# Setting the bound register of an indirect scatter before the semaphore wait, and waiting at the scatter itself

## The chip, the cores and the metric

The kernel runs on one core of one Trainium2 chip. The metric is the device time of one execution in microseconds (us). Its engines are PE (TensorE), DVE (VectorE), ACT (ScalarE), POOL (GpSimd) and SP (SyncE); each has a sequencer that reads its own list of instructions, written PEq, DVEq, ACTq, POOLq and SPq in the profile.

## What is computed

Three stages follow each other. The first is a linear attention with decay, the second an ELU network of 1536 tokens x 384 features with 2048 hidden units, the third a top-1 mixture of 8 experts with 384 places each. Cut to what matters:

```
x = attention(r, k, v, w, u)                 # 1536 x 384
h = x @ w_in; x = where(h > 0, h, exp(min(h, 0)) - 1) @ w_out
e = argmax(x @ w_gate); gate_w = softmax(x @ w_gate)[e]
disp[e, n_e] = x[i]                          # tokens sorted by expert
y = maximum(disp @ w1[e], 0) @ w2[e]
out[i] = gate_w[i] * y[e, n_e]               # back to the token's row
```

## The kernel before, in words

All products run on PE in fp32r, each value split into a high and a low part, so that one product is three matmuls (L1362 to L1364). ACT and DVE bring results out of the banks and form the parts; POOL forms many of the low parts (L707 for the ELU network's `g_lo`, L724 for half of each expert's weights).

Tokens are sorted by expert through memory. The ELU network works on 6 blocks (NB) of 256 tokens (two tiles of 128). When a block is done, DVE computes the slot number of each token (`slot_i`, L1150, which raises the semaphore `s_row`), and POOL writes the block's two tiles to the tensor `slots` with two indirect DMAs (`scatter_rows`, L681 to L685): 12 scatters in the whole run. They stand in POOL's list between the `g_lo` operations (L707) and the pieces of the attention that POOL works ahead on; the last two stand behind a wait for the first loads of the experts.

SP loads each expert's 256 rows back (`xrow`). An expert runs 8 steps on PE, and its output is two tiles of 128 tokens x 384, scaled by the gate on DVE (`yrow`, L1254 and L1314, which raise `s_ye`). `tok_i` (L1308, `s_tok`) holds the row of `out` to which each token goes. POOL sends each tile there with an indirect DMA (L729 in `scatter_tile`): 16 scatters, of which the first two, the next two (`scatter_out(0, 1)`), eight in a loop over the middle experts, and four behind the loop. The last expert's second tile is the last result of the run. Afterwards SP waits until all scatters have landed (L557), each engine reads a number that tells whether an expert had more than 256 tokens (L558, L758), and all engines meet (L177).

Of the kernel before, what the change touches and what calls it, by code (L numbers as in the profile page):

```python
# [12 lines left out]
def build(nc, B, H, S, D, DFF, NE, FE, CAP, rkt_in, nat_in, decay, bonus, bonus_pair, win, wout, wouttr, wgate, wexp, out, slots):  # L13
    T = B * S
# [44 lines left out]
    NSLOT = LATE + CAP  # L59
# [117 lines left out]
    with ctx:  # L177
# [13 lines left out]
        def pair(name):  # L191
            return [sem(f"{name}{p}") for p in range(2)]
# [88 lines left out]
        s_ye = pair("ye_ready")  # L281
        s_tok = pair("tok_ready")
# [292 lines left out]
        def _(pool):  # L575
# [98 lines left out]
            one = pool.alloc_register("one")  # L674
            last_slot = pool.alloc_register("last_slot")
            last_token = pool.alloc_register("last_token")
            pool.reg_mov(one, 1)

            def scatter_rows(n, t):

                pool.wait_ge(s_row, n + 1)  # L681
                pool.reg_add(last_slot, one, NSLOT - 2)  # L682
                nc.gpsimd.indirect_dma_start(
                    out=slots, out_offset=bass.IndirectOffsetOnAxis(ap=slot_i[n % 2][:, t:t + 1], axis=0),
                    in_=x2row[n % 2][:, t, NE:NE + XR], in_offset=None, bounds_check=last_slot, oob_is_err=False).then_inc(s_scat[n % 2], 16)  # L685
# [15 lines left out]
            for n in range(NB):  # L701
                for f in range(FT):
                    q = FT * n + f
                    if q == FT * NB - 1:
                        break
                    pool.wait_ge(s_ghi, q + 1)
                    nc.gpsimd.tensor_tensor(g_lo[:, f % 4, :], elu[:, f % 2, :], g_hi[:, f % 4, :].bitcast(F32),  # L707
                                            ALU.subtract).then_inc(s_glo, 1)
                    ahead(n, f)
                    at = f - route(n - 1)["scatter"]  # L710
                    if n and 0 <= at < BT:
                        if n == 1 and at == 0:
                            pool.wait_ge(s_blank, 16 * NBLANK)
                        scatter_rows(n - 1, at)
            pool.wait_ge(s_xr[0], 32)
            for t in range(BT):
                scatter_rows(NB - 1, t)

            def split_w2(e_i, r):

                for c in range(N1):
                    pool.wait_ge(s_ehi[r], 2 * N1 * e_i + N1 + c + 1)
                    cols = slice(W1 + c * ECH, W1 + (c + 1) * ECH)
                    nc.gpsimd.tensor_tensor(EL[r][:, cols], ER[r][:, cols], EH[r][:, cols].bitcast(F32),  # L724
                                            ALU.subtract).then_inc(s_elo2[r], 1)

            def scatter_tile(r, t):
                pool.reg_add(last_token, one, T - 2)  # L728
                nc.gpsimd.indirect_dma_start(  # L729
                    out=out, out_offset=bass.IndirectOffsetOnAxis(ap=tok_i[r][:, t, :], axis=0),  # L730
                    in_=yrow[r][:, t, :], in_offset=None, bounds_check=last_token,
                    oob_is_err=False).then_inc(s_sout[r], 16)

            def scatter_out(i, r):
                pool.wait_ge(s_tok[r], i + 1)
                for t in range(2):
                    pool.wait_ge(s_ye[r], 2 * i + t + 1)
                    scatter_tile(r, t)

            split_w2(0, 1)  # L740
            pool.wait_ge(s_atok, 1)
            pool.wait_ge(s_ye[0], 1)
            scatter_tile(0, 0)
            pool.wait_ge(s_tok[0], 1)
            pool.wait_ge(s_ye[0], 2)
            scatter_tile(0, 1)
            split_w2(1, 0)
            scatter_out(0, 1)
            with pool.Fori(1, NE // 2 - 1) as i:
                split_w2(i, 1)  # L750
                scatter_out(i, 0)
                split_w2(i + 1, 0)
                scatter_out(i, 1)
            split_w2(NE // 2 - 1, 1)
            scatter_out(NE // 2 - 1, 0)
            scatter_out(NE // 2 - 1, 1)
            pool.wait_ge(s_over, 1)
            over = pool.value_load(n_over[0:1, 0:1], min_val=0, max_val=T)  # L758
            with pool.If(over > SN):
# [1110 lines left out]
```

## Time and profile before

| | |
|---|---|
| median of 3 runs | 415.98 us |
| lowest and highest run | 415.86, 416.11 us |
| span of the profiled execution | 413.8 us |
| what lies around the span (median less span) | 2.1 us |
| PE busy | 406.2 us, 98% of the span |
| POOL busy | 231.0 us, 56% |
| DVE busy | 243.7 us, 59% |
| PE's share of the chain that ended last | 92% |
| POOL's share of it | 1% |

The profiled execution has no time of its own beside its span; what lies around the span is taken from the median. The span runs from the first to the last instruction. A row of the time line has its start, its duration and the instruction; in brackets stands how long the engine was idle before it, and what ended that. Instructions of a sequencer (a register, a semaphore wait, a branch) don't count as busy time and show in the chain of waits and in the view of their line, not in the time line of the engine.

### The profile page before, as it was taken

To read this page: it belongs to the slowest core of one execution; us is meant where nothing else is said; L and a number is where in the kernel's file an instruction comes from. 1 tells how busy PE (TensorE), PEld (TensorE's weight loads), DVE (VectorE), ACT (ScalarE), POOL (GpSimd) and SP (SyncE) were. 2 spreads that over 40 slices of the span, in tenths; PEclk is the share of its full clock that TensorE was granted. 3 is DMA by queue.
4 is the path that set the end of the run, shared out by engine and by line. 5 is a ranking of instruction groups with operands and counts; after the bars stand their busy time and mean duration, and the time that the engine had idled before them with its cause. 6 is when DMAs were issued, how large, how long until landed. Compare 5 with 4: busy or idle time off the path is not lost.

```text
span 413.8 us, 9451 instructions
## 1 busy us (share of the span) xinstructions
PE 406.2 (98%) x3697; PEld 390.8 (94%) x3697; DVE 243.7 (59%) x576; ACT 188.1 (45%) x409; POOL 231.0 (56%) x239
## 2 busy tenths in 40 slices
PE   8999999999999999999999999999999999999994
PEld 8799799999999999999999999999999999999994
DVE  7787955376576547654653487785635556364521
ACT  4786543233433333333343555553645445464420
POOL 3789775467856685668234336075073461825531
PEclk9999999999999999999999999999999999999999
DMA  7998996204030403020018001827383845729000
GB/s 287 402 396 351 367 344 243 82 38 148 12 119 2 139 21 118 3 86 21 2 20 344 2 2 38 326 77 248 125 308 101 340 160 203 295 89 360 5 31 28
DMA packets 18650, 64.98 MB, mean 157 GB/s; under 512 B 2203, under 2 KB 11717, under 8 KB 16432
## 3 DMA queue, kind: packets, MB, share of 16 engines
q1 hardware_dynamic: 16672, 59.67, 39.5%
q0 software_dynamic: 1792, 4.73, 3.0%
q8 instruction: 28, 0.46, 0.4%
q14 instruction: 14, 0.11, 0.1%
q10 hardware_dynamic: 144, 0.00, 0.0%
HBM read 51.98 MB, written 13.21 MB: 158 GB/s over the span
## 4 chain that ended last, share of the span: by engine, by line
PE 92%; DVE 4%; issue 1%; POOL 1%; ACT 1%; DMA 0%; POOLq 0%; DVEq 0%
PE bank L1362 27%; PE bank L1364 26%; PE bank L1363 26%; PE bank L1383 2%; PE bank L1412 1%; PE bank L1448 1%; PE bank L1452 1%; PE bank L1686 1%; PE bank L1441 1%; PE bank L1444 1%; PE bank L1539 1%; PE bank L1721 1%; PE bank L1722 1%; PE bank L1725 1%; PE bank L1625 1%
## 5 line engine op out<-in xcount | busy, mean ns | idle before, releaser
L707 POOL TENSOR_TENSOR g_lo<-elu,g_hi 128x256 fp32r<-128x256 f32 x95 | 73.8, 778 | 86.5 <-ACT g_hi L875 86.3
L1362 PE MATMUL bank<-xt,wd_hi 128*128 128x256 f32 x285 | 80.7, 283 | 0.6 <-DVE elu L1190 0.6
L1364 PE MATMUL bank<-xt,wd_lo 128*128 128x256 f32 x285 | 80.5, 282 | 0.0
L1363 PE MATMUL bank<-xt,wd_hi 128*128 128x256 f32 x285 | 80.4, 282 | 0.0
L866 ACT ACTIVATE elu<-elu 128x256 f32<-128x256 f32 x96 | 40.1, 418 | 76.5 <-DVE elu L1182 75.9
L1362 PE MATMUL bank<-wd_hi,g_hi 128*128 128x392 f32 (+1 forms) x192 | 67.5, 352 | 0.0
L1364 PE MATMUL bank<-wd_hi,g_lo 128*128 128x392 f32 (+1 forms) x192 | 65.3, 340 | 0.0
L1363 PE MATMUL bank<-wd_lo,g_hi 128*128 128x392 f32 (+1 forms) x192 | 65.2, 339 | 0.0
L1190 DVE SCALAR_TENSOR_TENSOR elu<-elu,bank 128x256 f32<-128x256 f32 x96 | 40.3, 420 | 40.5 <-ACT elu L866 40.5
L875 ACT CAST g_hi<-elu 128x256 fp32r<-128x256 f32 x96 | 39.0, 406 | 45.0 <-DVE elu L1190 45.0
L1362 PEld LDWEIGHTS bank<-xt,wd_hi 128*128 128x128 f32 x285 | 54.0, 189 | 1.3 <-DVE elu L1190 1.1
L1364 PEld LDWEIGHTS bank<-xt,wd_lo 128*128 128x128 f32 x285 | 54.2, 190 | 0.0
L1363 PEld LDWEIGHTS bank<-xt,wd_hi 128*128 128x128 f32 x285 | 54.1, 190 | 0.0
L1294 DVE SCALAR_TENSOR_TENSOR ge_lo<-bank,ge_hi 128x256 fp32r<-128x256 f32 x56 | 23.8, 425 | 48.8 <-ACT ge_hi L933 48.8
L1182 DVE TENSOR_SCALAR elu<-bank 128x256 f32<-128x256 f32 x80 | 33.8, 423 | 31.1 <-PE bank L1364 26.5
L933 ACT ACTIVATE ge_hi<-bank 128x256 fp32r<-128x256 f32 x56 | 21.6, 385 | 53.1 <-PE bank L1364 31.1
L724 POOL TENSOR_TENSOR wd_lo<-wd_raw,wd_hi 128x1024 fp32r<-128x1024 f32 x12 | 30.4, 2556 | 26.7 <-ACT wd_hi L946 24.3
L1362 PEld LDWEIGHTS bank<-wd_hi,g_hi 128*128 128x128 f32 x192 | 36.4, 189 | 2.0 <-issue 1.4
L1363 PEld LDWEIGHTS bank<-wd_lo,g_hi 128*128 128x128 f32 x192 | 36.4, 190 | 0.0
L724 POOL TENSOR_TENSOR we_lo<-we_raw,we_hi 128x1024 fp32r<-128x1024 f32 x9 | 21.3, 2398 | 26.9 <-ACT we_hi L946 26.9
L1364 PEld LDWEIGHTS bank<-wd_hi,g_lo 128*128 128x128 f32 x192 | 36.1, 188 | 0.0
L729 POOL DMA_INDIRECT out<-yrow,tok_i x16 | 15.7, 983 | 18.5 <-DVE yrow L1314 11.7
(220 smaller groups left out, 946.2 us busy)
## 6 DMA issues: line engine op xcount, KB each, us to landing
we_raw<-wexp SPq DMA_DIRECT2D x8, 1536.0 KB, 6.5
wd_raw<-wexp SPq DMA_DIRECT2D x8, 1536.0 KB, 7.7
rkt<-rkt SPq DMA_DIRECT2D x12, 512.0 KB, 5.5
nat<-nat SPq DMA_DIRECT2D x9, 672.0 KB, 5.0
xrow<-slots SPq DMA_DIRECT2D x16, 193.0 KB, 7.3
wd_raw<-win SPq DMA_DIRECT2D x4, 768.0 KB, 8.0
wd_raw<-wout SPq DMA_DIRECT2D x4, 768.0 KB, 8.9
wo_tr<-wouttr SPq DMA_DIRECT2D x1, 3072.0 KB, 17.8
```

The lines of the kernel that those rows point to most:

```text
L707: nc.gpsimd.tensor_tensor(g_lo[:, f % 4, :], elu[:, f % 2, :], g_hi[:, f % 4, :].bitcast(F32), ALU.subtract).then_inc(s_glo, 1)
L724: nc.gpsimd.tensor_tensor(EL[r][:, cols], ER[r][:, cols], EH[r][:, cols].bitcast(F32), ALU.subtract).then_inc(s_elo2[r], 1)
L729: nc.gpsimd.indirect_dma_start(out=out, out_offset=bass.IndirectOffsetOnAxis(ap=tok_i[r][:, t, :], axis=0), in_=yrow[r][:, t, :], in_offse ...
L866: nc.scalar.activation(elu[:, f % 2, :], elu[:, f % 2, :], ACT.Exp, scale=-1.0 if n == 0 else 1.0).then_inc(s_exp, 1)
L875: nc.scalar.copy(g_hi[:, f % 4, :], elu[:, f % 2, :]).then_inc(s_ghi, 1)
L933: nc.scalar.activation(ge_hi[:, f % 4, :], ps_e[f % 2][:, 0:SN], ACT.Relu).then_inc(s_gehi, 1)
L1182: V.tensor_scalar_min(elu[:, f % 2, :], ps_h[f % 2][:, 0:BN], 0.0).then_inc(s_m, 1)
L1190: V.scalar_tensor_tensor(out=elu[:, f % 2, :], in0=elu[:, f % 2, :], scalar=-1.0, in1=ps_h[f % 2][:, 0:BN], op0=ALU.add, op1=ALU.max).then ...
L1294: V.scalar_tensor_tensor(out=ge_lo[:, f % 4, :], in0=ps_e[f % 2][:, 0:SN], scalar=0.0, in1=ge_hi[:, f % 4, :].bitcast(F32), op0=ALU.max, o ...
L1362: mm(dst, w_hi, x_hi, start=start, stop=False)
L1363: mm(dst, w_hi, x_lo, start=False, stop=False)
L1364: return mm(dst, w_lo, x_hi, start=False, stop=stop)
```

## The change

For the twelve scatters of `scatter_rows` and for six of the sixteen scatters of `out` (the first two and the last four), `reg_add` is issued first, and the wait for the data comes behind it, so that it becomes part of the indirect DMA. A wait for another semaphore (`s_blank`, `s_xr`, `s_atok`, `s_tok`) that stood ahead stays ahead and becomes part of the `reg_add`. The other ten scatters (`scatter_out(0, 1)` and the loop) keep their order. The counts waited for are the same.

```diff
             def scatter_rows(n, t):
 
+                pool.reg_add(last_slot, one, NSLOT - 2)
                 pool.wait_ge(s_row, n + 1)
-                pool.reg_add(last_slot, one, NSLOT - 2)
                 nc.gpsimd.indirect_dma_start(
...
             def scatter_tile(r, t):
-                pool.reg_add(last_token, one, T - 2)
+
                 nc.gpsimd.indirect_dma_start(
...
                 for t in range(2):
                     pool.wait_ge(s_ye[r], 2 * i + t + 1)
+                    pool.reg_add(last_token, one, T - 2)
                     scatter_tile(r, t)
+
+            def scatter_now(r, t, count):
+
+                pool.reg_add(last_token, one, T - 2)
+                pool.wait_ge(s_ye[r], count)
+                scatter_tile(r, t)
 
             split_w2(0, 1)
             pool.wait_ge(s_atok, 1)
-            pool.wait_ge(s_ye[0], 1)
-            scatter_tile(0, 0)
+            scatter_now(0, 0, 1)
             pool.wait_ge(s_tok[0], 1)
-            pool.wait_ge(s_ye[0], 2)
-            scatter_tile(0, 1)
+            scatter_now(0, 1, 2)
             split_w2(1, 0)
             scatter_out(0, 1)
...
             split_w2(NE // 2 - 1, 1)
-            scatter_out(NE // 2 - 1, 0)
-            scatter_out(NE // 2 - 1, 1)
+            for r in range(2):
+                pool.wait_ge(s_tok[r], NE // 2)
+                for t in range(2):
+                    scatter_now(r, t, NE - 1 + t)
             pool.wait_ge(s_over, 1)
```

## Rows read from the trace of the kernel before

**Rows 1.** What PE waited for in the whole run, longest first.

```profile
PE bank L1466 <- DVE x2t L986: 1.1, 1, 1.1
PE bank L1362 <- DVE elu L1190: 0.6, 2, 0.3
PE bank L1441 <- DVE att L1031: 0.2, 1, 0.2
```

**Rows 2.** The chain that ended last, 407 to 411.5 us: start, us, what.

```profile
407.03 0.63 DVE yrow L1314
407.66 0.03 issue
407.69 0.02 POOLq L737
407.70 0.04 issue
407.75 0.03 POOLq L728
407.78 0.73 issue
408.51 0.77 POOL out L729
409.28 0.53 issue
409.81 0.77 POOLq L758
410.57 0.41 POOL out L729
```

**Rows 3.** Time line of DVE and POOL from 406 us to the end.

```profile
407.03 0.62 DVE L1314 TENSOR_SCALAR yrow<-bank,xrow 128x384 f32<-128x384 f32 x1 [1.25 <-PE bank L1364]
...
408.51 0.97 POOL L729 DMA_INDIRECT out<-yrow,tok_i  x1 [11.70 <-DVE yrow L1314]
408.60 0.62 DVE L1314 TENSOR_SCALAR yrow<-bank,xrow 128x384 f32<-128x384 f32 x1 [0.95 <-PE bank L1364]
410.01 0.97 POOL L729 DMA_INDIRECT out<-yrow,tok_i  x1 [0.53 <-issue]
```

**Rows 4.** Lines L728 and L758: the last bound register, the read of the overflow count.

```profile
L728 POOLq ALU_OP  x16: 32/32/32, 279.1 to 409.2; - x16
...
L758 POOLq TENSOR_LOAD <-n_over x1: 765/765/765, 409.8 to 409.8; - x1
```

**Rows 5.** Line L177, where the engines meet at the end: durations in ns, starts.

```profile
L177 POOLq EVENT_SEMAPHORE  x2: 17/17/17, 413.7 to 413.7; - x2
...
L177 POOLq DRAIN  x1: 2565/2565/2565, 411.0 to 411.0; - x1
L177 SPq DRAIN  x1: 7/7/7, 413.5 to 413.5; - x1
```

**Rows 6.** Time line, 219.1 to 220.7 us: a POOL operation with its own wait, then a scatter.

```profile
219.19 0.41 ACT L875 CAST g_hi<-elu 128x256 fp32r<-128x256 f32 x1 [0.49 <-DVE elu L1190]
219.67 0.74 POOL L707 TENSOR_TENSOR g_lo<-elu,g_hi 128x256 fp32r<-128x256 f32 x1 [3.20 <-ACT g_hi L875]
220.43 0.42 ACT L866 ACTIVATE elu<-elu 128x256 f32<-128x256 f32 x1 [0.84 <-DVE elu L1182]
220.57 1.03 POOL L683 DMA_INDIRECT slots<-x2row,slot_i  x1 [0.15 <-issue]
```

**Rows 7.** Time line of POOL, 390 to 398 us: two scatters behind each other.

```profile
394.53 0.99 POOL L729 DMA_INDIRECT out<-yrow,tok_i  x1 [0.16 <-issue]
395.83 0.97 POOL L729 DMA_INDIRECT out<-yrow,tok_i  x1 [0.30 <-issue]
```

**Rows 8.** Time line of POOL, 136 to 150 us: its fullest stretch around two scatters.

```profile
140.56 1.03 POOL L683 DMA_INDIRECT slots<-x2row,slot_i  x1 [0.15 <-issue]
141.62 0.74 POOL L707 TENSOR_TENSOR g_lo<-elu,g_hi 128x256 fp32r<-128x256 f32 x1
...
144.24 1.01 POOL L683 DMA_INDIRECT slots<-x2row,slot_i  x1 [0.17 <-issue]
```

**Rows 9.** Who waited for whom, 136 to 150 us: total us, times, longest.

```profile
DVE elu L1182 <- POOL g_lo L707: 1.7, 1, 1.7
```

**Rows 10.** Time line, 96 to 101.5 us: an SP load that carries its own wait.

```profile
97.18 0.62 PE L1452 MATMUL bank<-att,nat 128*32 128x128 f32 x16
...
97.89 0.33 SPq L459 DMA_DIRECT2D nat<-nat  x1
```

**Rows 11.** Line L683: the twelve scatters to slots, durations in ns, starts.

```profile
L683 POOL DMA_INDIRECT slots<-x2row,slot_i x12: 972/1003/1178, 96.0 to 270.4; - x12
its engine sat idle before it (us, times) until:
  DVE slot_i L1150: 8.6, 1
  issue: 3.0, 11
```

## The prediction

> **What bounds the kernel now.** I read the list of what PE waited for first, because PE is busy for 98% of the span. It waited 1.9 us in three places, the first of them at the start, and none of its waits is for POOL [rows 1]. A scatter that starts earlier in the middle of the run therefore gives PE nothing to do sooner. So the question is what happens behind PE's last matmul, where the chain leaves PE. The chain of waits of the last microseconds [rows 2] and the time line beside it [rows 3] show it: DVE scales the last expert's first tile (ends 407.65), POOL scatters it from 408.51; DVE scales the second tile (408.60 to 409.22), POOL scatters that from 410.01 to 410.98. The DMA then lands, SP and POOL close their lists, and the engines meet at 413.7 [rows 5]. The reader is to see two things. The second scatter isn't held by the first, which ended at 409.48 and left POOL idle for 0.53 us; it is held by the last tile's data. And from data ready (409.22) to scatter start (410.01) 0.79 us pass in which no engine computes.
>
> What fills these 0.79 us? The register instruction carries the wait; the last one starts at 409.2, and the chain goes on from its end at 409.28 [rows 2, 4], so the signal takes 0.03 us and the instruction 0.03 us. The sequencer's next instruction, behind the scatter in the list, is the read of the overflow count, and it starts at 409.81 [rows 2, 4]: the sequencer is busy with the scatter for 0.53 us. The scatter shows on the engine 0.20 us after that. The same holds for the tile before: register instruction done at 407.78, scatter at 408.51, 0.73 us = 0.53 + 0.20 [rows 2]. This 0.53 us of handling is paid behind the wait, because the wait stands one instruction ahead of it.
>
> **The change, part by part.** All is set against the profiled span of 413.8 us; with the 2.1 us around it that is the median of 415.98, to which I refer every time below. The three runs lie 0.25 us apart. I take 0.2%, 0.83 us, as what a measurement of this kernel can tell from no change, so from 415.15 to 416.81 is "the same".
>
> The last scatter. The register instruction now runs while POOL has nothing to do (0.03 us and the 0.03 us around it leave the path). Whether the 0.53 us of handling leave it too depends on whether the sequencer handles a scatter before or after the wait that the scatter itself carries. No scatter in this trace carries one, so I bound it. Lower end: the handling stays behind the wait; the gain is the register instruction and one fetch, 0.06 us. Upper end: the scatter sits ready, and starts as soon after the signal as any POOL operation that carries its own wait: g_lo starts 0.07 us after g_hi ended (219.60 to 219.67) [rows 6]. That would be a gain of 0.79 - 0.07 = 0.72 us. A scatter that is handled already still shows 0.15 us after the end of the operation before it, at 220.57 behind 220.41 [rows 6], and 0.16 behind an operation whose running time had covered the handling [rows 7]; so I take 0.07 + 0.15 = 0.22 us to 0.24, and a gain of 0.79 - 0.24 = 0.55 us. Of the two ends I take the one with the handling ahead, because the nearest rows in kind are POOL's own: an operation of the same engine with its own wait starts 0.07 us after the signal, and scatters behind a running operation have plainly been handled and queued while the engine was not free (0.16 us instead of 0.73).
>
> The Trainium skill says in "Perfetto Trace Analysis", DMA Instruction — SWDGE (GPSIMD), that the sequencer decodes such a DMA and pushes it into a wait queue, and that the semaphore is waited for there. By that rule the handling is ahead of the wait and the result is 415.43; were it not so, 415.92. No scatter of this trace carries a wait, so the trace neither confirms nor denies it.
>
> The scatter before it moves by the same 0.55 us or more (its two waits become one at the register instruction, and an EVENT_SEMAPHORE of 0.02 us with a fetch of 0.04 us goes too [rows 2]), to about 407.9. Scatters behind each other need 1.30 us from start to start (394.53 to 395.83) [rows 7]; 407.9 + 1.3 = 409.2 is before the 409.46 at which the last one now starts, so the next thing that could be late, POOL itself, isn't.
>
> Behind the last scatter everything hangs on it: its landing, which SP waits for, and POOL's drain of 2.57 us, begun at 411.0, just behind the scatter's end at 410.98, and ended at 413.6 [rows 3, 5]. POOL's read of the overflow count stands behind the scatter and moves with it, since it follows the handling; it must not become the last: it lasts 0.77 us, and 0.43 us pass from its end at 410.57 to the drain [rows 2, 5]; started when the scatter's wait is released (409.25), it would let the drain begin near 410.45, as the scatter does, which then ends at 410.43. So the end moves by the scatter's 0.55 us.
>
> The other scatters. The two ahead of the last expert's, ready long before the weights' low parts on POOL are done, start behind those parts at 394.53 and 395.83 [rows 7]; nothing changes. The first two of out (279 to 288 us) and the twelve of slots [rows 11] may start up to 0.55 us earlier where POOL waits for data. Eleven of the twelve were ready when POOL came to them (idle 3.0 us in all, 11 times), one waited 8.6 us for slot numbers [rows 11]. I cost them at nothing: PE covers them, as it waits for no result of POOL [rows 1]. The waits added to the scatters hold up what stands behind in POOL's list, as the waits at the register did; the order is the same, so nobody new is queued. No DMA is added or moved past another on SP.
>
> Sum: 415.98 - 0.55 = 415.43.
>
> **The rivals.**
>
 That no scatter of this trace carries a wait speaks for it a little.
>
> *Slower: scatters that are no longer handled under the operation before them.* If a scatter with its own wait were taken up only when POOL's earlier work is done, its 0.53 us would no longer be covered: it would start 0.73 us after the operation before it instead of 0.15. The place is 138 to 149 us and the like stretch of the next block, where POOL runs two scatters almost without a gap [rows 8] and DVE waits 1.7 us for a g_lo [rows 9]. Two scatters each, 4 x 0.58 = 2.3 us of lateness, and PE would feel what its lead doesn't cover. All of it gives 415.98 + 2.3 - 0.06 = 418.2. It decides from where some 0.9 us reach PE. Against it: the semaphore of these scatters is raised long before, so there is nothing to wait for, and PE has no wait there now.
>
> *More than forecast.* The scatter starts 0.07 us after the signal like g_lo, and the drain closes sooner than the scatter's shift. That is 0.72 us, 415.26, and to pass the bound of 0.83 it needs another 0.1 us.
>
> **How the numbers follow.** The forecast (handled ahead) gets 0.53, handled after 0.28, wait apart 0.10, slower 0.04, more 0.05. The forecast's own range is 415.3 to 415.6; the range that holds 8 in 10 must reach the second case with the spread of the runs, 0.1 us: 415.25 to 416.05. Only a gain above 0.83 us counts as faster. The forecast's 0.55 us does not, so faster gets 0.07 (most of "more", and a little of the first for an effect at the transition between stages), slower 0.04, the same 0.89.
>
> **What would show it.** In the changed profile the last scatter should start about 0.24 us behind the end of the last yrow and not 0.79; the last register instruction should stand before the last yrow's end; the time line up to 407 us should be the same within 0.1 us, PE's waits unchanged; POOL's drain should still last about 2.6 us. Rival one shows as a scatter 0.73 us behind the yrow, rival two as a new EVENT_SEMAPHORE just ahead of each scatter. Scatters that start 0.7 us behind a running operation would show the slower case. A shift of more than 0.2 us anywhere before 406 us would prove the reading wrong that PE covers the rest.

## The result, and the profile after

| | before | after |
|---|---|---|
| median of 21 runs each, same chip, in turn | 415.70 us | 415.09 us |
| lowest and highest of them | 414.90, 416.31 us | 414.40, 415.56 us |
| ratio, 95% interval | | 0.9986 [0.9979, 0.9992] |
| span of the profiled execution | 413.8 us | 413.7 us |

The changed kernel is faster by 0.6 us, between 0.3 and 0.9 by the interval. The forecast was a gain of 0.55 us; the forecast time, 415.43, was reckoned from the 415.98 of three runs. The measured 415.09 lies below the range (415.25 to 416.05). The gain stays under the 0.83 us that the prediction took as what a measurement can tell from no change; 21 runs of each kernel did tell 0.6 us from none. The kernel before measured 415.70 here, and 415.69, 416.18 and 416.08 us beside the experiments (21 runs each).

The spans of the two profiles differ by only 0.1 us: the profiled run of the changed kernel took 415.56 us, the longest of its 21. So they are compared from the last yrow on. The time line of DVE and POOL after, which answers to [rows 3]:

```profile
407.47 0.62 DVE L1321 TENSOR_SCALAR yrow<-bank,xrow 128x384 f32<-128x384 f32 x1 [1.25 <-PE bank L1371]
408.36 0.97 POOL L729 DMA_INDIRECT out<-yrow,tok_i  x1 [11.10 <-DVE yrow L1321]
409.03 0.62 DVE L1321 TENSOR_SCALAR yrow<-bank,xrow 128x384 f32<-128x384 f32 x1 [0.94 <-PE bank L1371]
409.93 0.97 POOL L729 DMA_INDIRECT out<-yrow,tok_i  x1 [0.59 <-DVE yrow L1321]
```

The last yrow ends at 409.65, its scatter starts at 409.93: 0.28 us, where it was 0.79 by the rounded rows of [rows 3] and 0.80 by the trace's nanoseconds. Count the rest from that yrow too. Before, the span of 413.85 us ended 4.63 us behind it (409.22); now the span of 413.75 us ends 4.10 us behind it (409.65). That is the gain, 0.53 us, as the difference of one number from each trace. The profile now names the yrow as what the last scatter waited for; in [rows 3] it said "issue", because the sequencer was at work.

The chain of waits after, which answers to [rows 2]:

```profile
402.16 5.96 issue
408.13 0.03 POOLq L743
408.16 0.20 issue
408.36 0.97 POOL out L729
409.33 0.36 issue
409.69 0.78 POOLq L765
```

Look at the sequencer's own instructions. The bound for the first tile is set by 402.16, nearly 6 us before that tile is there. The bound for the last tile (L743) is set at 408.13, 0.04 us after the first tile's yrow ended at 408.09, and the read of the overflow count (L765) starts at 409.69, 0.04 us after the last yrow ended. So the sequencer handles one scatter ahead and goes no further than that scatter's wait; what stands behind comes when the wait is released. (Behind these scatters stand instructions of the sequencer itself, a register operation and a read; what it would do with a second scatter or a computation there was not tried.) The handling of the last scatter has no row of its own. With the 0.53 us of before it would run from 408.16 to some 408.7, an estimate, while DVE has nothing yet to scale.

Where the engines meet, which answers to [rows 5]:

```profile
L177 POOLq DRAIN  x1: 2574/2574/2574, 410.9 to 410.9; - x1
L177 SPq DRAIN  x1: 7/7/7, 413.4 to 413.4; - x1
```

And what PE's weight loads waited for, in the kernel before and then in the kernel after. These two answers were not among the rows of the prediction, and they matter below:

```profile
PEld bank L1362 <- issue: 1.6, 5, 0.8
...
PEld bank L1412 <- POOL nat L624: 0.3, 1, 0.3
...
PEld bank L1686 <- DMA xrow<-slots: 0.2, 1, 0.2
```

```profile
PEld bank L1369 <- POOL g_lo L707: 0.8, 1, 0.8
...
PEld bank L1693 <- DMA xrow<-slots: 0.6, 2, 0.4
```

### The profile page after: what moved, and what is told of

Read it like the earlier page. It is cut to its first block, busy times and chain, and to the rows that moved or that the text cites. A ratio compares the mean times of both kernels' runs of the same rounds, so it can differ in the third digit from the quotient of the medians.

```text
span 413.7 us, 9445 instructions
## 1 busy us (share of the span) xinstructions
PE 406.2 (98%) x3697; PEld 390.3 (94%) x3697; DVE 242.4 (59%) x576; ACT 188.1 (45%) x409; POOL 231.4 (56%) x239
## 4 chain that ended last, share of the span: by engine, by line
PE 88%; DVE 4%; issue 3%; DMA 3%; POOL 1%; ACT 1%; POOLq 0%; SPq 0%; DVEq 0%
PE bank L1369 26%; PE bank L1371 25%; PE bank L1370 24%; PE bank L1390 2%; DMA xrow<-slots 2%; PE bank L1419 1%; PE bank L1455 1%; PE bank L1459 1%; PE bank L1693 1%; PE bank L1448 1%; PE bank L1451 1%; PE bank L1546 1%; PE bank L1728 1%; PE bank L1729 1%; PE bank L1632 1%
```

## The experiments

Where a kernel was timed, it stands beside 21 runs of the kernel before on the same chip, 11 runs of its own. "Gap" is from the end of the last yrow to the start of the last scatter.

### The very last scatter alone

```diff
-            scatter_out(NE // 2 - 1, 1)
+            pool.wait_ge(s_tok[1], NE // 2)
+            pool.wait_ge(s_ye[1], NE - 1)
+            scatter_tile(1, 0)                       # the old order
+            pool.reg_add(last_token, one, T - 2)
+            pool.wait_ge(s_ye[1], NE)                # the new order
+            nc.gpsimd.indirect_dma_start(...)
```

> The kernel before, with the new order for the very last scatter alone; the other 27 keep the old one. Theory (the whole gain is the 0.5 us of handling that leaves the path behind the last yrow): the last scatter starts 0.27 us behind the end of the last yrow, as in the changed kernel, instead of 0.79, and the time is 0.5 us below before (ratio 0.9987). Rival (part of the 0.6 us measured comes from scatters in the middle of the run): the gap is 0.27 us too, but the time falls by less than 0.3 us.

Measured: 415.44 us against 415.69, ratio 0.9993 [0.9984, 1.0002]. Neither expectation had the gap right, for it is 0.57 us. The time line shows why:

```profile
407.26 0.62 DVE L1322 TENSOR_SCALAR yrow<-bank,xrow 128x384 f32<-128x384 f32 x1 [1.25 <-PE bank L1372]
408.74 0.97 POOL L729 DMA_INDIRECT out<-yrow,tok_i  x1 [11.74 <-DVE yrow L1322]
408.82 0.62 DVE L1322 TENSOR_SCALAR yrow<-bank,xrow 128x384 f32<-128x384 f32 x1 [0.94 <-PE bank L1372]
410.01 0.97 POOL L761 DMA_INDIRECT out<-yrow,tok_i  x1 [0.30 <-issue]
```

The scatter before it, in the old order, starts at 408.74, and the last one comes 1.27 us behind it, 0.30 us after its end: the spacing that [rows 7] showed for two scatters in a row. The last scatter had been handled, and POOL wasn't free. It gains 0.23 us, no more: the span ends 4.40 us behind the last yrow instead of 4.63. The medians differ by 0.25 us, which fits, but the interval holds 1, so the time alone shows nothing. The new order pays in full only if both scatters of the last expert have it.

### All scatters but the last

```diff
                 for t in range(2):
-                    scatter_now(r, t, NE - 1 + t)
+                    if r and t:
+                        pool.wait_ge(s_ye[r], NE)
+                        pool.reg_add(last_token, one, T - 2)
+                        scatter_tile(r, t)
+                    else:
+                        scatter_now(r, t, NE - 1 + t)
```

> The changed kernel, with the old order for the very last scatter alone. Theory: the last scatter starts 0.79 us behind the last yrow again, the time is that of before within 0.2 us (ratio 1.000), though 17 scatters keep the new order. Rival (the middle of the run gives part of it): 0.2 us or more below before.

Measured: 415.69 us against 415.69, ratio 1.000 [0.9991, 1.0009]; gap 0.80 us, span end 4.64 us behind the last yrow. The chain of waits again has the handling behind the register instruction, for this scatter alone:

```profile
409.31 0.03 POOLq L765
409.35 0.52 issue
409.87 0.50 POOLq L770
```

With 17 of the 18 scatters in the new order nothing is gained. The middle of the run gives nothing that this measurement, good to some 0.4 us, can see; the time lines compared in the part on the prediction say it more sharply.

### The last expert's two scatters alone

```diff
-            scatter_out(NE // 2 - 1, 1)
+            pool.wait_ge(s_tok[1], NE // 2)
+            for t in range(2):
+                pool.reg_add(last_token, one, T - 2)
+                pool.wait_ge(s_ye[1], NE - 1 + t)
+                nc.gpsimd.indirect_dma_start(...)
```

> The kernel before, with the new order for the last expert's two scatters; the other 26 keep the old one. Theory (the gain sits behind the last yrow, and both scatters must move, since two scatters keep 1.27 to 1.30 us from start to start): the last scatter starts 0.27 us behind the last yrow, the first one 0.27 us behind its own, and the time is 0.5 us below before (ratio 0.9987), the whole effect of the change. Rival (the other 16 scatters have a part in it): less than 0.35 us below before, with the same gaps.

Measured: 415.57 us against 416.18, ratio 0.9984 [0.9975, 0.9993]; both gaps 0.28 us, span end 4.11 us behind the last yrow. Two of the 28 scatters bring the whole effect of the change.

### A second register operation between wait and scatter: a miss

```diff
                     pool.reg_add(last_token, one, T - 2)
                     pool.wait_ge(s_ye[r], NE - 1 + t)
+                    pool.reg_add(other_reg, one, T - 2)
                     scatter_tile(r, t)
```

> The changed kernel, where for the last four scatters a second register operation, on a register that nobody reads, stands between the wait and the scatter, so the wait falls to it and the scatter carries none; the bound register is set long before. Theory (the handling is done before the wait only if the scatter itself carries the wait): the last scatter starts 0.79 us behind the last yrow. Rival (what costs is reading a register just written): 0.3 us, since the bound is set long before.

The gap is 0.28 us, as if the rival were right. It says nothing: the trace has no such instruction. The operation on `other_reg`, which nobody reads, never came into the list that POOL runs, so this was the changed kernel again (415.28 us, one run).

### Ten register operations behind the wait: the same miss

```diff
+                        pool.reg_add(last_token, one, T - 2)
+                        pool.wait_ge(s_ye[r], NE)
+                        for _ in range(10):
+                            pool.reg_add(other_reg, one, T - 2)
+                        scatter_tile(r, t)
```

> The changed kernel, with ten operations on an unread register between the last wait and the last scatter. Theory: the ten take 0.06 us each and the handling of 0.53 us follows them, so the last scatter starts 0.73 + 10 x 0.06 = 1.3 to 1.4 us behind the last yrow, and the end moves with it by 1.1 us against the changed kernel. Rival (the tail is bounded by something beside the scatter, the drain or the reads of the count): the scatter moves by 1.1 us, the end by less.

The ten are missing from the trace too; gap 0.28 us (415.70 us, one run). Both questions were asked again, with waits and with a read, which do stand in the trace.

### Which of two waits the scatter carries

The two kernels have the same instructions in POOL's list. They differ in the order of two waits, for the last expert's scatters; `s_over` has been there for over 100 us.

```diff
                     pool.reg_add(last_token, one, T - 2)
                     pool.wait_ge(s_ye[r], NE - 1 + t)
+                    pool.wait_ge(s_over, 1)          # one kernel: second; the other: first
                     scatter_tile(r, t)
```

> The changed kernel; the last expert's two scatters wait for the yrow and then for a semaphore that has long been there (the overflow count's). One wait rides on the scatter, the other becomes an instruction of its own ahead of it. Theory (what counts is that the data's wait rides on the scatter): where the trace shows the yrow's semaphore at the scatter, it starts 0.27 us behind the yrow; where the trace shows it at the EVENT_SEMAPHORE ahead, 0.79 us, although the bound register is set long before and no register operation stands between. Rival (a register just written costs the time): 0.27 to 0.33 us in both.

> As the kernel with the count's wait second, with the two waits in the other order in the source, so that the other one of them rides on the scatter. Theory: of the two kernels one shows a gap of 0.27 us and the other 0.79 us, by which wait rides; the ends of the spans, counted from the last yrow's end, differ by the same 0.5 us. Rival (register): no difference.

The view of the line of the second wait (an EVENT_SEMAPHORE of its own), with `s_over` second and then with `s_over` first:

```profile
L766 POOLq EVENT_SEMAPHORE  x2: 17/17/17, 402.2 to 408.2; - x2
```

```profile
L766 POOLq EVENT_SEMAPHORE  x2: 17/17/17, 408.6 to 410.2; - x2
```

The wait written first rides on the scatter, the one written second becomes the instruction ahead. With `s_over` second, that instruction passes at once (402.2 and 408.2) and the scatter carries the data's wait: gap 0.28 us. With `s_over` first, the EVENT_SEMAPHORE waits for the data (last yrow ends at 410.18, it runs at 410.21), and the gap is 0.78 us:

```profile
409.56 0.62 DVE L1327 TENSOR_SCALAR yrow<-bank,xrow 128x384 f32<-128x384 f32 x1 [0.95 <-PE bank L1377]
410.96 0.97 POOL L729 DMA_INDIRECT out<-yrow,tok_i  x1 [0.59 <-issue]
```

The bound register is set before the data's wait in both, and no register operation stands between wait and scatter in either. So it isn't the register that costs the half microsecond. It is whether the data's wait stands at the scatter. Counted from the last yrow, the spans end 4.11 and 4.62 us behind. (415.49 and 416.64 us, one run each. Of the 1.15 us between them 0.51 lie behind the last yrow; another 0.50 come from PE, which reached it that much later in the second profile, and 0.14 lie outside the spans.)

### The reads of the overflow count moved ahead

```diff
+            pool.wait_ge(s_over, 1)
+            over = pool.value_load(n_over[0:1, 0:1], min_val=0, max_val=T)
             for r in range(2):                        # the last four scatters
...
-            pool.wait_ge(s_over, 1)
-            over = pool.value_load(n_over[0:1, 0:1], min_val=0, max_val=T)
```

and on SP likewise, ahead of its wait for the landings.

> The changed kernel, with the reads of the overflow count moved ahead: on POOL ahead of the last four scatters, on SP ahead of its wait for the landings. Theory (the end hangs on the last scatter: POOL's drain ends 2.62 us behind the last scatter's end, 1.20 us behind the last landing, in five of five traces, whenever it began): no gain, the time is that of the changed kernel, 0.5 us below before, though the drain begins some 0.5 to 1 us earlier. Rival (the sequencer's work behind the last scatter holds the end): 0.4 to 1.0 us below the changed kernel, 1.0 us or more below before.

Measured: 415.72 us against 416.18, ratio 0.9985 [0.9976, 0.9994], the gain of the changed kernel and nothing on top. Line L177 of this kernel, and its last scatter:

```profile
L177 POOLq DRAIN  x1: 3658/3658/3658, 410.3 to 410.3; - x1
L177 SPq DRAIN  x1: 7/7/7, 413.0 to 413.0; - x1
```

```profile
410.33 0.97 POOL L729 DMA_INDIRECT out<-yrow,tok_i  x1 [0.59 <-DVE yrow L1321]
```

SP is done at 413.0, 1.0 us ahead of the meeting at 414.0, and POOL's drain begins at 410.3, before the scatter itself. It takes 1.08 us more (3.66 instead of 2.57) and ends, as in every other profile, 2.6 us behind the scatter's end (411.31 to 413.93) and 1.20 us behind its landing (412.74). The span ends 4.11 us behind the last yrow. The drain follows the scatter and its landing; no reading of the count is on the path.

### The read between wait and scatter

```diff
+                        pool.reg_add(last_token, one, T - 2)
+                        pool.wait_ge(s_ye[r], NE)
+                        over = pool.value_load(n_over[0:1, 0:1], min_val=0, max_val=T)
+                        scatter_tile(r, t)            # for r = t = 1
```

> The changed kernel, with POOL's read of the overflow count moved between the wait for the last yrow and the last scatter, so that the read carries the wait and the scatter none. Theory (sequencer work behind the wait counts in full, and the handling of the scatter follows it): the last scatter starts about 0.03 + 0.5 to 0.8 (read) + 0.75 = 1.3 to 1.8 us behind the last yrow, and the span's end moves back by the same 1.0 to 1.5 us against the changed kernel, to 5.1 to 5.6 us behind the last yrow. Rival (the drain bounds the end by itself): the end moves by less than the scatter.

```profile
409.25 0.62 DVE L1325 TENSOR_SCALAR yrow<-bank,xrow 128x384 f32<-128x384 f32 x1 [0.95 <-PE bank L1375]
411.67 0.97 POOL L729 DMA_INDIRECT out<-yrow,tok_i  x1 [2.12 <-issue]
```

Gap 1.81 us (409.86 to 411.67), 1.53 us more than in the changed kernel; the span of 415.51 us ends 5.65 us behind the yrow, 1.54 us more (417.32 us, one run). Both stand just above what was expected, because the read is three instructions (start 409.9, end 410.93) and costs 1.03 us:

```profile
L766 POOLq TENSOR_LOAD <-n_over x1: 774/774/774, 409.9 to 409.9; - x1
L766 POOLq FUSED_REGOPS  x1: 168/168/168, 410.7 to 410.7; - x1
L766 POOLq SEQ_ASSERT  x1: 28/28/28, 410.9 to 410.9; - x1
```

The 1.81 us are 0.04 for the signal, 1.03 for the read, and 0.74 from there to the scatter, as behind a register instruction that carries the wait (0.73). What stands between the wait and the scatter comes back in full at the end, and so does the handling.

### The changed kernel once more

> The changed kernel once more, beside the kernel before on the same chip. Theory (the gap behind the last yrow is fixed, what moves from run to run is when PE gets there): the ratio is 0.9987 again within its interval, the last scatter starts 0.28 us behind the last yrow and the span ends 4.10 us behind it, to 0.02 us, while the end of the last yrow itself lies anywhere within some 0.8 us. Rival (the tail itself varies): the 4.10 us differ by 0.1 us or more from the first profile.

Measured: 415.57 us against 416.08, ratio 0.9985 [0.9976, 0.9994]; gap 0.28 us, span end 4.11 us behind the last yrow. The yrow itself ends at 409.93, 0.28 us later than in the first profile of the same kernel.

### Rows ahead of weights

```diff
-                    sp.wait_ge(s_fc2e, ET * (2 * i + r + 1))
-                    load_w2(2 * i + 2 + r, r)
                     sp.wait_ge(s_ye[r], 2 * (i + 1))
                     sp.wait_ge(s_tok[r], i + 1)
                     load_x(2 * i + 2 + r, r)
+                    sp.wait_ge(s_fc2e, ET * (2 * i + r + 1))
+                    load_w2(2 * i + 2 + r, r)
```

> The changed kernel, where SP loads an expert's rows ahead of the second part of its weights. PE's weight loads waited 0.2 to 0.8 us for xrow in the expert stage, once or twice a run, a part of what differs from run to run. One theory (the rows queue behind 1.5 MB of weights): these waits go, PE gets to the last yrow 0.2 to 0.6 us earlier, 0.2 to 0.6 us below the changed kernel. Rival (the weights' second part, for which ACT already waited 1.0 to 1.4 us once, comes 1 to 2 us later and reaches PE): same or up to 2 us slower than the changed kernel.

Measured: 415.34 us against 416.08 of the kernel before, ratio 0.9980 [0.9971, 0.9989], and against 415.57 of the changed kernel beside it. The view of the matmuls and weight loads of line L1693, which take xrow in, has this for the changed kernel in that job:

```profile
its engine sat idle before it (us, times) until:
  DMA xrow<-slots: 0.9, 2
```

and no such wait for this kernel. The two profiles stand 0.06 us apart at 318 us (one and the same `ge_hi` of ACT starts at 318.33 and 318.39), and the last yrow ends at 409.93 and 409.47, earlier with the rows first. Its 11 runs lie within 0.25 us (415.24 to 415.49), those of the changed kernel within 0.58 (415.19 to 415.77). The two intervals against the kernel before overlap, so that it is faster than the changed kernel, by 0.23 us, is suggested and not shown. Its ratio to the kernel before is the lowest measured, and the interval leaves no doubt that it is faster than that kernel.

## Why the prediction came out as it did

**The mechanism was right.** It was the case given a chance of 0.53: the sequencer handles a scatter before the wait that the scatter carries. The pair of kernels with swapped waits shows it, 0.28 against 0.78 us, and throws out "handled after the wait". It also throws out "the change does not do what it says": in the changed kernel's trace no EVENT_SEMAPHORE stands between the last two register operations and their scatters. The rule of the Trainium skill in "Perfetto Trace Analysis", DMA Instruction — SWDGE (GPSIMD), is borne out here as far as times can show it: decoding and pushing come ahead of the semaphore's wait (gap 0.28 us with the wait at the scatter, 0.78 with it one instruction ahead).

**The size.** The term 0.79 - 0.24 = 0.55 us measured 0.79 - 0.28 = 0.51 us by the rounded rows, 0.52 unrounded, and 0.53 us where the spans' ends are counted from the last yrow. The estimate of the start behind the signal, 0.07 us like g_lo plus 0.15 like a queued scatter, was 0.04 to 0.06 us short. The 0.61 us between the medians, 0.3 to 0.9 by the interval, agree with both.

**What failed is the level, and with it the range.** The mis-sized term of "Sum: 415.98 - 0.55 = 415.43" is the first: the 415.98 of three runs measured 415.70 beside the changed kernel, 0.28 us lower, and that is most of the 0.34 us by which the time missed the forecast. The step that made the range too narrow was: "the range that holds 8 in 10 must reach the second case with the spread of the runs, 0.1 us". It took three runs that lie 0.25 us apart for the spread of the kernel. Over 84 runs in four sets of 21 the same kernel before took 414.90 to 416.75 us, and its medians by set were 415.69 to 416.18. A low end 0.18 us below the forecast does not cover that. 415.09 is where this gain leads when the kernel before stands at 415.70.

A part of the level can be seen in the profiles. In the seven of the two sets with the higher medians (416.18 and 416.08) PE's work falls 0.3 to 0.4 us behind between 96 and 98 us, in the other six it doesn't: `elu` on ACT starts at 95.32 us in the kernel before and at 95.37 in the second profile of the changed kernel, PE's first matmul of the next `wd_hi`, `g_hi` group at 97.73 and 98.08. The profile names no releaser for that wait ("issue"), so its cause stays open. The step is about as large as the difference between the sets' medians (0.4 to 0.5 us), but that it makes this difference is not shown: the kernel before was profiled in none of the four sets.

**A view that was not read.** "It waited 1.9 us in three places, ... and none of its waits is for POOL" was read from PE's matmuls alone; the weight loads have a list of their own, shown above, and in the kernel before it names POOL's `nat` with 0.3 us. They waited for xrow, between nothing and 0.8 us in the twelve profiles with the weights first (0.2 in the kernel before), and 0.84 us for a g_lo at 48 us. The g_lo wait is in all thirteen profiles with the same length, in the kernel before as "issue", so it isn't the change's. The xrow wait is a part of what moves PE's arrival from run to run; loading the rows first removed it in the one profile taken. The rest are steps in the first 110 us, whose cause was not tried.

**"The time line up to 407 us should be the same within 0.1 us"** was therefore the wrong test. The last yrow ended 0.43 us later in the changed profile, and two profiles of one and the same kernel differ by 0.28 us there. By its own words the prediction would have called its reading wrong. What answers the question is where the 0.43 us arise. The same `elu` on ACT starts at 19.16 in the kernel before and at 19.32 in the changed one, ahead of any scatter; the same `ge_hi`, behind all twelve scatters of slots, starts at 317.99 and 318.12. So from 19 to 318 us the distance stays at 0.16 to 0.13 us, and the rest comes at 332 and 385 us, where PE's weight loads waited 0.2 and 0.4 us for xrow (before, 0.2 us at 385 alone). PE covered the scatters in between, though five of them started 0.4 to 0.6 us earlier: the first two of slots (96.00 to 95.40, 98.13 to 97.76), the last two of slots (269.13 to 268.69, 270.43 to 269.99) and the second of out (287.39 to 286.94). The first of slots had been late for its data, too (POOL's idle time ahead of it fell from 1.27 to 0.52 us), where the prediction counted eleven of twelve as ready. The kernel with all scatters but the last in the new order, at ratio 1.000, agrees that the middle of the run has no part in the gain.

**"The second scatter isn't held by the first"** was true of the kernel before, and true of the changed one (409.33 to 409.93 idle). The arithmetic with 1.30 us from start to start was needed all the same: with the last scatter alone moved, the first one does hold it.

**The tail behind the scatter** moved as forecast: the drain lasted 2.57 us in both. The slower case didn't come up: the scatters behind a running operation still start 0.15 us after it (140.71 after 140.56).

## What to carry to other kernels

Read which instruction carries a wait: sequencer work between the wait and a slow-to-handle instruction counts in full when the data is late, so set registers first and let the data's wait be the one that rides on the DMA (with two waits, the one written first rode in these kernels). Two such DMAs in a row keep a distance, 1.27 to 1.30 us from start to start here, so move them together. For a change of half a microsecond, count both traces from the last common event before the edit, and take level and spread from many runs in several sets, not from three.

## What the runs showed of the hardware that was not expected

- The sequencer handles one waiting scatter ahead and stops there: a register instruction behind it runs 0.03 to 0.04 us after that scatter's wait is released (408.13 behind 408.09), though it needs nothing. Behind the last scatter a read and, in the kernel with the reads moved ahead, a branch do the same.
- POOL's drain ends 2.6 us behind the last scatter's end, and 1.20 us behind its landing to within 0.01 us in all thirteen profiles, whether it begins at 410.9 or at 410.3, 0.06 us before the scatter starts.
- From the data to the recorded start of a scatter that was handled ahead 0.28 us pass, the same to 0.01 us in the eight profiles where both of the last two scatters carried the data's wait, for either of them.
- The register operations whose result nobody reads were missing from the traces of both kernels that had them; they are no use as a dose.
